# Weight splits on POOL: one instruction a head from head 4, or whole groups in heads 8 to 14

## The reference, cut to what matters

```
# 1: attention, 4 batches x 8 heads = 32 heads, 1152 keys, 576 pooled queries, 64 columns
q_pool = q.reshape(B, H, S // 2, 2, D).mean(axis=3)
scores = q_pool @ k.transpose(0, 1, 3, 2) / sqrt(D)
attn = exp(scores - max(scores)); attn = attn / (sum(attn) + 1e-09)
x = attn @ v
# 2: for each of 4 experts e, on x of each batch
q, k, v = x @ wq[e], x @ wk[e], x @ wv[e]
ye = softmax(causal(q @ k.T / sqrt(64))) @ v @ wo[e]     # mixed by the gates of x @ w_gate
# 3: u = x + (x.T @ U @ V).T ; out = u + relu(u @ w_ch1) @ w_ch2
```

## Time and profile before

| | |
|---|---|
| median of three runs | 1178.35 us (1176.79 to 1178.52) |
| the profiled execution | 1178.35 us, its span 1176.6 us |
| busy in the span | PE 1120.3, PEld 928.5, DVE 810.7, ACT 620.0, POOL 686.5 us |
| instructions | 19898 |
| granted PE clock, share of full | 0.992 |
| first and last exponential of attention (L574) | 22.6 and 518.9 us |

### The profile page before, as it was taken

One profiled execution on the slowest core, in us unless ns is written; L12 is line 12 of the kernel. 1 busy time (PEld: TensorE's weight loads), 2 busy tenths in 40 slices (PEclk: granted clock), 3 DMA queues, 4 the chain that ended last, 5 costly groups with the idle time before them and its releaser, 6 DMA issues. The chain is left out here.

```text
span 1176.6 us, 19898 instructions
## 1 busy us (share of the span) xinstructions
PE 1120.3 (95%) x7088; PEld 928.5 (79%) x7088; DVE 810.7 (69%) x1573; ACT 620.0 (53%) x1228; POOL 686.5 (58%) x689
## 2 busy tenths in 40 slices
PE   6999999999999999997899989779999999999998
PEld 5877778777777777786778777568888888888897
DVE  5788888888888888857556565655548754686554
ACT  4666666666666566546565656633334333443331
POOL 5888989989899899734333425422344333633330
PEclk9999999999999999999999999999999999999999
DMA  8211122222222121001001012132122512223121
GB/s 208 62 59 51 47 59 62 61 61 62 62 61 62 32 61 41 22 6 32 2 1 42 1 36 75 43 118 86 53 72 68 171 55 67 72 77 105 56 68 54
DMA packets 76593, 71.47 MB, mean 61 GB/s; under 512 B 11856, under 2 KB 54864, under 8 KB 76496
## 3 DMA queue, kind: packets, MB, share of 16 engines
q1 hardware_dynamic: 75888, 69.90, 19.9%
q10 hardware_dynamic: 608, 0.30, 0.1%
HBM read 60.74 MB, written 9.44 MB: 60 GB/s over the span
## 5 line engine op out<-in xcount | busy, mean ns | idle before, releaser
L645 DVE TENSOR_REDUCE part_max<-psA 128x1 f32<-128x384 f32 x465 | 250.4, 556 | 58.3 <-PE psA L380 35.5
L574 ACT ACTIVATE pT<-psA 128x576 f32<-128x576 f32 x288 | 187.6, 652 | 159.1 <-PE psA L399 150.4
L271 POOL TENSOR_TENSOR pT<-pT 128x576 f32<-128x576 f32 x157 | 222.6, 1418 | 25.7 <-ACT pT L574 3.6
L2156 DVE TENSOR_TENSOR hidden_parts<-psC,hidden_parts 128x384 f32<-128x384 f32 x168 | 91.0, 554 | 129.2 <-PE psC L2004 119.6
L380 PE MATMUL psA<-kT,qT 128*128 128x384 f32 x465 | 165.6, 378 | 5.2 <-DVE part_max L645 4.7
L413 PE MATMUL psA<-pT,v_raw 128*64 128x288 f32 x1152 | 153.8, 412 | 0.0
L1829 POOL TENSOR_TENSOR w_raw<-w_raw 128x256 f32<-128x256 f32 x24 | 17.7, 736 | 215.0 <-DMA w_raw<-in_moe_w_ch 214.8
L390 PE MATMUL psA<-qT,kT 128*128 128x288 f32 x576 | 132.4, 311 | 0.0
L399 PE MATMUL psA<-qTm,kT 128*128 128x288 f32 x576 | 123.2, 295 | 0.5 <-ACT qTm L560 0.5
L413 PEld LDWEIGHTS psA<-pT,v_raw 128*64 128x64 f32 x1152 | 76.9, 136 | 53.2 <-issue 6.3
L390 PEld LDWEIGHTS psA<-qT,kT 128*128 128x128 f32 x576 | 98.5, 189 | 18.4 <-issue 14.0
(11 more groups left out here) (197 smaller groups left out, 2632.4 us busy)
## 6 DMA issues: line engine op xcount, KB each, us to landing
w_raw<-in_moe_w_ch SPq DMA_DIRECT2D x48, 256.0 KB, 3.1
k_raw<-in_k SPq DMA_DIRECT2D x32, 288.0 KB, 3.1
v_raw<-in_v SPq DMA_DIRECT2D x32, 288.0 KB, 2.8
q_raw<-in_q SPq DMA_DIRECT2D x31, 256.0 KB, 3.3
w_even<-in_moe_w_ch SPq DMA_DIRECT2D x12, 512.0 KB, 5.0
w_odd<-in_moe_w_ch SPq DMA_DIRECT2D x12, 512.0 KB, 4.9
u_rows<-x_all SPq DMA_DIRECT2D x16, 256.0 KB, 2.0
u_even<-u_rows SPq DMA_DIRECT2D x2, 1536.0 KB, 6.8
```

Of the source, the lines that this page charges most:

```text
L271: nc.gpsimd.tensor_tensor(pT[:, KT, :], pT[:, KT, :], pT[:, j, :], ALU.add).then_inc(part_summed, 1)
L574: nc.scalar.activation(pT[:, j, :].rearrange("p (a c) -> p a c", a=2), scores[n % 2][:, :, 0:HALF], ACT.Exp, scale=0.5 * float(D) ** -0.5) ...
L645: nc.vector.tensor_reduce(part_max[u][:, t, c:c + 1], maxes[n % 2][:, 0:PIECE], AX.X, ALU.max).then_inc(max_freed[n % 2], 1)
L2156: nc.vector.tensor_tensor(to, session((k, n))[:, 0:W], other, ALU.add).then_inc(added, 1)
```

## The change

The 26 weight splits are issued in other heads. Heads 4 to 7 and 15 to 29 carry none. Heads 8 to 11 carry the four instructions of one expert each, heads 12 and 13 the four of a half of wv, gate and wo, head 14 the two of V. All of them still stand behind the adds of their head on POOL. Inside a group an instruction waits only for those whose result it reads. The wait for the weights' landing moves from head 4 to head 8, and the wait for all 26 from the end of the loop to head 14. The other engines' programs keep their instructions and their order.

```
-    SPLIT_FROM = 4
+    SPLIT_FROM = 8
...
-                if SPLIT_FROM <= h < SPLIT_FROM + ready.SPLITS:
-                    ready.split(pool, h - SPLIT_FROM)
-            pool.wait_ge(ready.w_split, ready.SPLITS)
+                if SPLIT_FROM <= h < SPLIT_FROM + ready.E:
+                    ready.split_expert(pool, h - SPLIT_FROM)
+                if h in (SPLIT_FROM + ready.E, SPLIT_FROM + ready.E + 1):
+                    ready.split_values(pool, h - SPLIT_FROM - ready.E)
+                if h == SPLIT_FROM + ready.E + 2:
+                    ready.split_V(pool)
...
+    def split_expert(self, pool, e):
+        ops, done, n = self.nc.gpsimd, self.w_split, 4 * e
+        if e == 0:
+            pool.wait_ge(self.w_loaded, 16 * self.LOADS)
+        else:
+            pool.wait_ge(done, n)
+        raw, hi, lo = (w[:, :, e, :] for w in (self.wqk_raw, *self.wqk))
+        ops.tensor_scalar(raw[:, :, 0:self.HD], raw[:, :, 0:self.HD], float(self.HD) ** -0.5,
+                          None, ALU.mult).then_inc(done, 1)
+        ops.tensor_copy(hi[:, :, self.HD:], raw[:, :, self.HD:]).then_inc(done, 1)
+        pool.wait_ge(done, n + 1)
+        ops.tensor_copy(hi[:, :, 0:self.HD], raw[:, :, 0:self.HD]).then_inc(done, 1)
+        pool.wait_ge(done, n + 3)
+        split_lo(ops, lo, raw, hi).then_inc(done, 1)
+
+    def split_values(self, pool, n):
+        ops, done, at = self.nc.gpsimd, self.w_split, 4 * self.E + 4 * n
+        pool.wait_ge(done, at)
+        raw, hi, lo = (w[:, 2 * n:2 * n + 2, :] for w in (self.wvg_raw, *self.wvg))
+        ops.tensor_copy(hi, raw).then_inc(done, 1)
+        out, out_hi, out_lo = (w[:, n, :] for w in (self.wo_raw, *self.wo_s))
+        ops.tensor_copy(out_hi, out).then_inc(done, 1)
+        pool.wait_ge(done, at + 2)
+        split_lo(ops, lo, raw, hi).then_inc(done, 1)
+        split_lo(ops, out_lo, out, out_hi).then_inc(done, 1)
```

More of the change, by code:

```diff
@@ L834, in load_weights @@
                          ).then_inc(loaded, 16)
-    def split(self, pool, n):
-        ops, done, E, HD = self.nc.gpsimd, self.w_split, self.E, self.HD
-        if n == 0:
+    def split_expert(self, pool, e):
+        ops, done, n = self.nc.gpsimd, self.w_split, 4 * e
+        if e == 0:
             pool.wait_ge(self.w_loaded, 16 * self.LOADS)
@@ L842, in split @@
             pool.wait_ge(done, n)
[L843 to L872, removed]
@@ L873, in split @@
-        ins.then_inc(done, 1)
+        raw, hi, lo = (w[:, :, e, :] for w in (self.wqk_raw, *self.wqk))
[5 more added lines that the diff above has]
+        pool.wait_ge(done, n + 3)
@@ L875, with split_V @@
+    def split_V(self, pool):
+        ops, done, at = self.nc.gpsimd, self.w_split, 4 * self.E + 8
+        pool.wait_ge(done, at)
+        ops.tensor_copy(self.V4[0][:, :], self.V4_raw[:, :]).then_inc(done, 1)
+        pool.wait_ge(done, at + 1)
+        split_lo(ops, self.V4[1][:, :], self.V4_raw[:, :], self.V4[0][:, :]).then_inc(done, 1)
+        pool.wait_ge(done, at + 2)
     SPLITS = 26
```

## The result

The changed kernel takes 1186.23 us (median of five, 1184.57 to 1188.42), the kernel before 1178.52 in the same runs (1176.79 to 1179.41). The forecast was 1186.2. The profiled execution of the changed kernel took 1188.16 us with a span of 1186.4, which is 1.9 us above the median.

What follows compares the result with a forecast made beforehand. PE bounds attention, delayed when POOL's late adds hold up DVE. Splits 25.1 plus stalls 3.5 less slack 7 x 1.93 make POOL 15.1 late, PE 14.5; less 6.7 removed, +7.8 on 1178.35 gives 1186.2 us, range 1181.5 to 1195.

Steps and rivals of the forecast that it cites:

- PE takes POOL's lateness less 0.9, and up to 1.2 more in head 15: Attention: POOL 15.1 us late makes PE 14.2 late, plus up to 1.2 from key split shutting out L671; taken as 14.5.
- Slack of 1.93 us a head: POOL in a quiet attention head: 13.37 us of work in a 15.30 us period; seven heads' slack subtracted from its lateness.
- The port's price: DVE and POOL lock a shared port; unhindered splits are shorter than recorded: 25.1 us in sum against 34.7.
- Rival 1: Recorded split durations hold, no lock gain: splits 34.7 us, net +13.6, 1192, or +18, 1196, with stalls; 20%.
- Sum of the splits, 25.1 us: POOL, heads 8 to 14: expert groups 13.8 us, values groups 8.6, V 2.8, less rounding.
- Stalls of the adds at DVE's first sum, 0.5 a head, 3.5: POOL's adds meet L666 in heads 9 to 15, costing 0.5 us more each, 3.5 us in all.
- Removed: 6.7 us: Heads 4 to 29 before: one split each cost 404.52 against 397.8 us, 6.7 us, all of it to go.
- Net of the attention stage, +7.8: Attention: PE's lateness of 14.5 less the removed 6.7, so 7.8 us longer.
- The rest keeps its length: Stages after attention: same instructions in the same order, so no change in length.
- Rival 2: No change that can be told: splits cost 19.9 us, up to 23.4 with stalls; net -1.2 to +2.3, 1177 to 1181; 8%.
- Rival 4: Attention without stalls at L666, else as summed: +4.0 us, 1182.4; low end of the main case, no separate chance.
- Rival 3: Faster: POOL's lateness never reaches PE, periods stay 15.3 with L671 late; only the 6.7 us gain remains, 1171.7; 6%.

Runs made afterwards that it cites:

- the floor: Kernel before without weight splits on POOL: ACT makes the hi parts, plain copies replace the lo parts, subtraction left out; 1172.04 us, ratio 0.9931.
- groups in every other head, repeated: Changed kernel, groups in heads 8, 10, ... 20, plus a key-split wait put one turn too early, already fulfilled; 1187.71 us.
- behind the query split: Kernel before, still one split a head, one head later, behind the query split instead of the adds; 1185.33 us, ratio 1.0040.
- every other head, key split waits: Changed kernel, groups in heads 8, 10, ... 20, POOL waiting for L671 before the key split behind the late adds; 1182.70 us.
- two a head: Kernel before with two splits a head in heads 4 to 16 instead of one in 4 to 29; ratio 1.0021.
- before again: Kernel before, unchanged, profiled a second time; 1180.25 us.
- every other head: Changed kernel with its seven groups in heads 8, 10, ... 20 instead of 8 to 14; 1195.2 us, ratio 1.0118.
- experts grouped: Part of the change: four expert groups in heads 8 to 11, the other ten splits one a head in heads 12 to 21; 1183.12 us.
- hi on ACT, lo in thirds: Kernel before with hi parts and scaling on ACT, lo parts in 27 thirds on POOL, one a head, behind the query split; 1174.75 us, ratio 0.9945.
- changed, key split waits in head 16: Changed kernel with POOL waiting for DVE's L671 before its key split, in turn 16 only; 1187.13 us.
- changed again: Changed kernel, unchanged, profiled a second time; 1189.02 us.

## Why the prediction was right

The mechanism was right, and runs show it; that the time came out at 1186.23 against 1186.2 was luck. The cost in attention was forecast 2.2 us too high, and a lengthening elsewhere, of 2 to 3 us, was put at nothing. By its own steps:

- **PE takes POOL's lateness less 0.9, and up to 1.2 more in head 15**: right. POOL's key split behind the adds of head 15 starts at 278.36, the first of the splits in head 8 at 159.28: 119.08 - 7 x 15.30 = 12.0 us late. 12.0 - 0.9 + 1.2 = 12.3, and PE lost 12.25. The 1.2 is shown by the run that takes it away, and the 0.9 by the same run: 12.0 - 0.9 = 11.1 was left. But I had taken 0.3 of the 1.2 into the 14.5, and so this term was 0.9 too low.
- **Slack of 1.93 us a head**: nearly right. Without the splits and the stalls POOL's seven turns take 119.08 - 23.4 - 2.7 = 93.0 us, 13.28 each, a slack of 2.02. Over seven heads that is 0.6 us less lateness.
- **The port's price**: right. L44 at 1.28, L846 at 0.84, casts at 0.40 to 0.47. Rival 1, the recorded durations, is out. What is said at the start, that the engines meet only at semaphores, is thus too narrow: DVE and POOL meet at the port too, and their busy times contain waits there. The Trainium skill's rule that I named there (in "SBUF — State Buffer", "SBUF: two separate sides") holds in these rows: 1.43 us of key split make 1.2 us more of L671. One kind does not fit it, see the last section.
- **Sum of the splits, 25.1 us**: too high by 1.7. From L846 to L237 the expert groups take 3.44, 2.93, 2.92 and 2.93 us, the values groups 4.26 and 4.27, V 2.64: 23.4. I charged every expert head 0.5 for a cast shut out by L671. Only the first head paid such a stall, and there L846 paid it to L668; in the next three DVE's sum started 0.05 to 0.06 us behind L846, took 0.95, and the casts came through.
- **Stalls of the adds at DVE's first sum, 0.5 a head, 3.5**: from L264 to the next instruction the adds take 9.48 to 9.72 us, 9.16 in a quiet head, and so 0.3 to 0.6 more, in sum 2.7.
- **Removed: 6.7 us**: 6.6 by the floor (404.5 - 397.9); 7.2 by the second profile of the kernel before.
- **Net of the attention stage, +7.8**: 410.16 - 404.52 = 5.6 us, or 5.0 from the second profile of each kernel. This is the mis-sized term, by 2.2 us: 1.7 for the splits, 0.8 for the stalls and 0.6 for the slack too high, 0.9 for head 15 too low.
- **"The rest keeps its length"**: not so. The difference of the medians is 7.7 us, and so 2 to 3 of it lie outside the stretch. In the first pair of profiles 3.3 us lie behind head 30, and 0.9 ahead of head 4, where the 13 profiles scatter by 1.7 us (96.4 to 98.1). What the rest goes with stands below.

The rest goes with the number of falls of PE's clock to 1.2 GHz in it. Each lasts 3.4 us by the records of the granted clock; a stretch of 6.8 us is counted as two, and those behind PE's last instruction are left out.

| falls in the rest | rest us | profiles |
|---|---|---|
| 3 | 673.9 | groups in every other head, repeated |
| 4 | 675.3 to 676.8 | before; behind the query split; every other head, key split waits; two a head |
| 5 | 676.7 to 678.5 | before again; changed; every other head; experts grouped |
| 6 | 679.1 to 679.7 | no splits on POOL; hi on ACT, lo in thirds; changed, key split waits in head 16 |
| 7 | 680.4 | changed again |

That is some 1.6 us a fall, whatever the kernel. The two kernels that reach the second stage 12 to 13 us earlier than the changed one (no splits on POOL, and hi on ACT) have six falls. So the longer rest does not come from the splits' lateness as such. Whether the moment at which the second stage begins sets the number of falls, or it only scatters (4 and 5 in the kernel before, 5 and 7 in the changed one), these runs do not settle. Why 2 to 3 us of the difference of the medians lie outside the stretch thus stays open.

Rival 2 needed the splits to cost about 21 with their stalls; they cost 26.1. Rival 4 had no stalls at the first sum; they are 2.7 us. Rival 3's one condition, a late L671 in a period of 15.3, was met in no head.

Of the signs that I named, these came out otherwise. The periods of heads 9 to 12 are 16.3 to 16.8 us and not 17 to 18. PE's own wait for part_max in the stretch of heads 4 to 30 went from 4.5 to 9.1 us, and that of its weight loads (PEld), which is the same pause seen by them, from 11.6 to 15.7, not up by 14. The attention stage ends 6.5 us later in the profiles and not 8.

## What to carry to other kernels

An instruction put on a side engine costs what it makes late, not what it lasts: find the instruction behind which the bound engine queues (here one sum on DVE), measure the side engine's slack up to it in one period, and spend no more than that in any single period. Where two engines share a port, look who starts some hundredths of a microsecond ahead, for that decides who pays, and a wait that makes the side engine later can be a gain. Filler that exceeds the slack is dearer spread out than in consecutive periods only as long as each gap lets the next instruction collide anew (14.5 against 12.3 us for the same seven groups). With the collision taken away by a wait it is the other way round, about 7.9 us spread out against 11.1 in consecutive heads, since each gap then refunds slack.

## What the hardware showed beyond that

In all three profiles of the changed kernel's order PE's clock fell to 1.2 GHz in the same head, 13 (19.35, 19.29 and 19.34 us). Four heads in which PE had been idle for 0.8 to 1.2 us each stood before it, and then one pause of 2.42 us, which ended 1.2 us ahead of the fall (at 248.6 us):

```profile
247.39 0.44 PE L382 MATMUL psA<-kT,qT 128*128 128x384 f32 x1 [2.42 <-DVE part_max L647]
```

The four heads alone do not do it: the kernel with only the experts grouped has the same four (16.31 to 16.80 us, PE idle for 0.7 to 1.2), no such pause behind them, and no fall. In the kernel before the clock never fell between heads 4 and 30. In the kernel with one split a head behind the query split PE was idle for 1.65 us in a head of 17.17, with two or three shorter heads before the next of that length, and it did not fall there either; with groups in every other head and idle times of 1.7 to 1.8 us in heads 9 and 11 it fell in head 13.

In the changed kernel the fall cost nothing, since POOL set the pace: POOL waited for no other engine meanwhile, the nine periods still sum to what POOL's own time gives, and the sum repeated within 0.1 us. In the kernel with groups in every other head, where PE set the pace again at once, each fall cost 1.5 us. So groups that make PE pause can cost twice, by the pause and by the clock behind it.

The scaling (L846, a tensor_scalar in place) does not hold the port for its whole time; here the rule named above does not fit. At 209.53 it started 0.06 us ahead of DVE's second sum and took 0.85 us; the sum lost 0.19 us (0.95 for 0.76), where a cast of 0.62 us cost it 0.38 (1.14 in heads 12 and 13). So the sum ended at 210.54, and the cast that started at 210.33 lost only 0.07 us (0.47 for 0.40); by my estimate a sum held up until shortly before L846's end, like those behind a cast, would have run to about 211.0 and shut it out.
